# A fused attention and two-layer mixer: TensorE's order inside a slot, the first block sums and the place of w_in's loads

## What is computed

```python
# q, k, v: (2, 8, 768, 64) float32; block 32, window 16
k_sum = k.reshape(B, H, nb, block, D).max(axis=3)
v_sum = v.reshape(B, H, nb, block, D).mean(axis=3)
scores_l = scale * q @ k.T, kept where |i - j| < window, else -1e9
scores_s = scale * q @ k_sum.T + log(block)
a = softmax(concat(scores_l, scores_s))
x = a @ concat(v, v_sum)                 # (2, 768, 512) after the heads are joined
h = relu(x @ w_in); u, v = halves of h; v = layer norm of v
x = (u * (w_spatial @ v + b)) @ w_out    # then the second mixer, with a convolution and a gate
```

## Time and profile before

| | us |
|---|---|
| median of 3 runs | 348.29 |
| lowest, highest | 347.79, 354.48 |
| profiled execution, its own time | 351.07 |
| profiled execution, its span | 349.1 |
| PE busy in the span | 337.3 |

### The profile page before, as it was taken

One profiled execution on the slowest core, in us unless ns is written; L12 is line 12 of the kernel. 1 busy time (PEld: TensorE's weight loads), 2 busy tenths in 40 slices (PEclk: granted clock), 3 DMA queues, 4 the chain that ended last, 5 costly groups with the idle time before them and its releaser, 6 DMA issues.

```text
span 349.1 us, 7117 instructions
## 1 busy us (share of the span) xinstructions
PE 337.3 (97%) x2890; PEld 303.3 (87%) x2890; DVE 211.4 (61%) x503; ACT 123.6 (35%) x364; POOL 117.5 (34%) x130
## 2 busy tenths in 40 slices
PE   8868899999999999999999999999999999999996
PEld 7657788888998899889999999998989999999984
DVE  5656788534308990354446984688656667766652
ACT  3656878656233132351111124231222232222212
POOL 6637768766609999400004930000000000000000
PEclk9989999999999999999999999999999999999999
DMA  8997849000212300163000100000000004000004
GB/s 251 282 262 190 279 112 323 7 2 3 62 60 70 116 11 2 45 200 118 0 0 2 60 0 3 0 2 0 0 2 0 0 2 180 0 2 0 0 3 180
DMA packets 9025, 24.72 MB, mean 71 GB/s; under 512 B 1185, under 2 KB 1185, under 8 KB 8993
## 3 DMA queue, kind: packets, MB, share of 16 engines
q1 hardware_dynamic: 8992, 24.26, 22.8%
HBM read 21.11 MB, written 3.15 MB: 69 GB/s over the span
## 4 chain that ended last, share of the span: by engine, by line
PE 91%; DMA 5%; SPq 2%; issue 1%; DVE 0%; DVEq 0%
PE bank L799 26%; PE bank L801 26%; PE bank L800 26%; PE bank L791 4%; DMA vw<-in_vw 4%; PE bank L778 3%; PE bank L758 3%; PE bank L849 2%; PE bank L768 1%; PE bank L852 1%; SPq L282 1%; DMA out<-obuf 1%; SPq L276 0%; DVE obuf L702 0%; SPq L271 0%
## 5 line engine op out<-in xcount | busy, mean ns | idle before, releaser
L801 PE MATMUL bank<-g_h,W_l 128*128 128x384 f32 x128 | 43.0, 336 | 0.0
L800 PE MATMUL bank<-g_l,W_h 128*128 128x384 f32 x128 | 43.0, 336 | 0.0
L799 PE MATMUL bank<-g_h,W_h 128*128 128x384 f32 x128 | 42.9, 335 | 0.0
L505 ACT ACTIVATE P<-P,nmax 128x120 f32<-128x120 f32 x96 | 36.7, 384 | 15.5 <-DVE nmax L634 15.4
L800 PE MATMUL bank<-wo_l,hg_h 128*128 128x512 f32 x96 | 38.0, 396 | 0.0
L801 PE MATMUL bank<-wo_h,hg_l 128*128 128x512 f32 x96 | 38.0, 396 | 0.0
L799 PE MATMUL bank<-wo_h,hg_h 128*128 128x512 f32 x96 | 38.0, 395 | 0.0
L421 POOL TENSOR_TENSOR P<-P,rinv 128x480 f32<-128x480 f32 x24 | 23.6, 986 | 26.1 <-DVE rinv L622 25.7
L801 PE MATMUL bank<-wsT_h,vn_l 128*128 128x384 f32 x96 | 32.1, 334 | 0.0
L799 PE MATMUL bank<-wsT_h,vn_h 128*128 128x384 f32 x96 | 32.1, 334 | 0.0
L800 PE MATMUL bank<-wsT_l,vn_h 128*128 128x384 f32 x96 | 32.1, 334 | 0.0
(11 more groups left out here) (111 smaller groups left out, 796.6 us busy)
## 6 DMA issues: line engine op xcount, KB each, us to landing
vw<-in_vw SPq DMA_DIRECT2D x16, 288.0 KB, 6.5
kT<-in_k SPq DMA_DIRECT2D x8, 384.0 KB, 5.1
qT<-in_q SPq DMA_DIRECT2D x8, 384.0 KB, 6.2
out<-obuf SPq DMA_DIRECT2D x12, 256.0 KB, 2.0
stage<-in_wsT SPq DMA_DIRECT2D x6, 384.0 KB, 3.1
stage<-in_w SPq DMA_DIRECT2D x4, 512.0 KB, 3.5
stage<-in_wo SPq DMA_DIRECT2D x4, 512.0 KB, 3.6
wi_most<-in_w_in SPq DMA_DIRECT2D x3, 512.0 KB, 12.9
```

The lines of the kernel that those rows point to most:

```text
L505: a.activation(P[:, i % NP_, j, :], P[:, i % NP_, j, :], ACT.Exp, bias=nmax[:, c:c + 1], scale=-1.0, accum_out=rsum[:, c, 0:1]).then_inc(e ...
L799: t_.matmul(dst, lhs[0](c), rhs[0](c), start=first, stop=False)
L800: t_.matmul(dst, lhs[0](c), rhs[1](c), start=False, stop=False)
L801: ins = t_.matmul(dst, lhs[1](c), rhs[0](c), start=False, stop=last)
```

## The change

In each slot, TensorE's transposes and values move ahead of the fills and of the identity transposes; the identity transposes of slot 0 go from 10 to 6. The block sums of pair 0 move one slot forward, "vs" from slot 1 to 0 and "vp" from 2 to 1, and `spread_sums(0)` on GpSimd moves from behind the normalization of item 1 to behind that of item 0. Pair 1 keeps slots 3 and 4, and all later pairs keep theirs. SyncE issues `vw` of a pair ahead of the quarter of w_in, not behind it. The orders on VectorE and ScalarE stay, but for the takes of pair 0's sums, which go with their fills.

```diff
@@ -177,7 +177,7 @@
         for p in range(NP):
-            at = GP * p - 1 if p >= 2 else 2 * p + 1
+            at = GP * p - 1 if p >= 2 else 3 * p
             fills_at[at].append(("vs", p))
             fills_at[at + 1].append(("vp", p))
@@ -298,9 +298,9 @@
             for p in range(NP):
                 load_k(p)
                 load_q(p)
+                load_v(p)
                 if 2 <= p < 2 + KC:
                     load_wi(p - 2)
-                load_v(p)
@@ -388,7 +388,7 @@
-                pool.wait_ge(norm_done, GP * p + 1 if p >= 2 else GP * p + 2)
+                pool.wait_ge(norm_done, GP * p + 2 if p == 1 else GP * p + 1)
@@ -420,7 +420,7 @@
-                if i in (2, 5) or i >= 2 * GP and i % GP == 1:
+                if i in (1, 5) or i >= 2 * GP and i % GP == 1:
                     spread_sums(i // GP)
@@ -880,17 +880,17 @@
             for i in range(SLOTS):
                 if i < NG:
                     scores(i)
+                if 2 <= i < NG + 2:
+                    transpose_probs(i - 2)
+                if 3 <= i < NG + 3:
+                    values(i - 3)
+                for _ in range(6 if i == 0 else 4 if i < 3 else 0 if i > 7 or any(u[0] == "vs" for u in fills_at[i]) else 3):
+                    t_.transpose(bank[1][:, 0:128], ident[:, :], ident[:, :])
                 for u in fills_at[i]:
                     if u[0] == "piece":
                         piece(*u[1:])
                     else:
                         dense(u)
-                for _ in range(10 if i == 0 else 4 if i < 3 else 0 if i > 7 or any(u[0] == "vs" for u in fills_at[i]) else 3):
-                    t_.transpose(bank[1][:, 0:128], ident[:, :], ident[:, :])
-                if 2 <= i < NG + 2:
-                    transpose_probs(i - 2)
-                if 3 <= i < NG + 3:
-                    values(i - 3)
```

## The result

The changed kernel takes 356.15 us (median of 4 runs, 354.83 to 359.3) against 349.0 us for the kernel before: ratio 1.0177, 95% interval 1.0121 to 1.0234. The ratios are estimated from the single executions without the slower state of the chip, so they are not quotients of the medians. It is slower, by 5 to 6 us going by the ratios (the medians lie 7.15 and 4.69 us apart); whether that is more than 2% the intervals leave open. The forecast was slower by 3.35 us, 351.6 us in a range of 347.4 to 354.0. The profiled execution of the changed kernel has a span of 357.3 us against 349.1, and it is one of the longer ones (its own time is 359.3).

A forecast was written before the change was run, and what follows sets the result against it. The prediction took TensorE (PE), 91% of the chain, as the bound. Waits on ACT's copies of 0.7 + 2.0 + 1.55 us less 0.9 in the front gave +3.35 on 348.3: 351.6 us, range 347.4 to 354.0.

The forecast's parts named there:

- the front: Before slot 12: more PE work done ahead of each instruction block boundary, so slot 12 starts 0.9 us earlier.
- ACT's late copy in slots 20, 23 and 26: PE waits for ACT's copy behind a dense tile's take: 1.0 us in slots 20 and 23, 1.55 in 26.
- slots 14 and 17: PE's transposes wait for ACT's copy of the transposed probabilities, 0.35 us in each slot, 0.7 us together.
- The work is the same, only what stands where a block ends differs.: Early slots: reordering leaves PE's work equal and changes only the work left behind the last block boundary, gaining 0.9 us.
- Fetch gaps behind slot 12: From 44 us on PE crosses instruction block boundaries without idle time, so no loss was put there.
- The wait for `vw`: Pair 2's block sums: vw lands about 1.9 us earlier, near 19 us, so the 1.06 us wait goes.
- a start of slot 12 before 42 us: Sign that the reading of instruction fetches setting the front's pace fails; slot 12 was expected near 43.3 us.
- The gaps were forecast longer than before: Front: "issue" gaps stay 124 matmuls apart and grow, as PE does more before each boundary and then stands longer.
- The first sums: Pair 0's sums moved to slot 0: costed at 0, with bounds of 1.25 us gain and 1.0 us loss.
- rival 4: The clock falls at the new waits on ACT: one fall 353.1 us, three (slots 20, 23, 26) 356.1; chance 0.18.
- Rival 3: The waits on ACT do not show because ACT is ahead by then: 347.4 us; chance 0.07.
- Rival 2: The front opens: early fetch gaps vanish and the clock stays high, 345.9 us, or 349.2 for half; chance 0.2.

The follow-up runs named there:

- e5: Changed kernel with the loads of the second layers' weights held until item 19's scores are done: 356.32 us against 351.54 for the kernel before.
- e4: Changed kernel with ScalarE's copy of the transposed probabilities ahead of x_h and, in slots 20, 23, 26, the dense tile's take: 353.77 us, ratio 1.0070 to the kernel before.
- e14: Changed kernel with the second layers' weight loads held back, run once more for a second trace; the traced execution took 357.10 us.
- e12: Kernel before with one more identity transpose ahead of the four transposes of slots 8 to 17: one execution, 351.76 us against 350.52.
- e13: Kernel before with one more identity transpose behind the values of slots 8 to 17, ahead of the next scores: one execution, 353.56 us against 350.52.
- e8: Changed kernel run again, unaltered, beside the kernel before on another chip: 355.94 against 351.25 us, ratio 1.0149.
- e6: Changed kernel with the values moved back to the end of the slot (scores, transposes, fills, values): 349.15 us, ratio 0.9912 to the kernel before.
- e9: Changed kernel with values last in the slot and ScalarE's copy ahead of x_h and the last dense tile: 347.85 us, ratio 0.9894 to the kernel before.
- e11: Same as e10, with the four loads of w_in one pair later (pairs 3 to 6) and its split one step later: 347.75 us, ratio 0.9897 to the kernel before.
- e10: Same as e9, with the first block sums back in slots 1 and 2 and ten identity transposes in slot 0: 347.36 us, ratio 0.9886 to the kernel before.
- e7: Kernel before with only the loads changed, vw ahead of w_in in SyncE's queue: 349.29 us against 351.54, ratio 0.9916.

## Why the prediction failed

**Direction and first cause were right.** The order costs more than the front gives, by ACT's late copy in slots 20, 23 and 26. Forecast 1.0, 1.0 and 1.55 us, measured as idle time 0.85, 0.85 and 1.34. The idle time says a little too little: at slot 20 the transposes start 1.61 us behind the scores, forecast 1.67, and slot 20 takes 6.53 us in e5 and 5.62 in e4, which has no wait, 0.91. In slots 14 and 17 0.35 us each were forecast; e14, which has no gap there, shows 2.86 and 2.85 us against 2.68 for both, 0.18 each. All of ACT's late copies together: forecast 4.25, measured 3.6 us (e5 and e14 against e4).

**The step that failed is the sentence "The work is the same, only what stands where a block ends differs."** The work was the same, but what stands next to what was not: one more change of kind in each slot that ends with a piece or a dense tile and is followed by scores (12, 13, 15, 16, 18 to 22), 0.16 us by e12 and e13. The forecast has no term for it; e4 measures 1.26 us from slot 12 on. The forecast's sum for the late part, 4.25 us, came near the measured 4.85 only by luck, because its waits were 0.65 us too large. So this term alone does not explain the miss. Going by the ratios the loss was 5.2 to 6.2 us, 1.9 to 2.8 over the forecast: 0.6 of it is the late part, 0.7 the front, and the rest fits the fetch gaps behind slot 12. The next two points take up the front and the gaps.

**The front gave next to nothing,** the second term that failed: -0.9 us forecast, -0.2 in the trace after and a start of slot 12 later than before in e8 and e14 (44.94 and 45.48 us). The wait for `vw` went, as forecast, and the next gap took it over. The 0.9 us rested on the blocks arriving when they had; in the seventeen traces of the two kernels and the variants slot 12 starts between 40.45 and 46.14 us: they don't arrive at fixed times. The forecast took a start of slot 12 before 42 us as a sign that fetches do not set the front's pace. It came in four traces (e5, e6, e9, e11), but these have 0 to 2.06 us of fetch gaps in the front against 4.04 before, so it fits fetches that come out differently from one execution to the next and does not speak against them. The gaps were forecast longer than before; in the trace after the front holds 2.85 us of them, and the new waits and the low clock in slot 8 take the difference. The first sums were costed at nothing with a loss of 1.0 us as a bound; they brought a wait of 0.95 us on POOL at 15.78, by `spread_sums(0)` ahead of the second normalization, which the forecast named and priced at nothing. The scores of slot 4 start at 17.77 us, 1.24 later than before, so the delay was not covered by the block awaited at 15.92 us: VectorE's copy, for which `values(0)` waits too, ended at 15.39 there, as this row of the kernel before shows, and that left room for 0.5 us.

```profile
14.70 0.69 DVE L602 COPY pT<-bank 120x512 f32<-120x512 f32 x1 [0.60 <-PE bank L778]
```

The time of e9 and e10 doesn't differ for it.

**Fetch gaps behind slot 12 were put at nothing**, the third term that failed: 1.89 us in the trace after, and with the last of them the clock fell, which costs 0.5 us in slot 17 (sums 1.33 us against 0.79) and about 1.0 in slot 18 (5.37 against 4.22 with 0.15 of it for the change of kind). That is rival 4 by another cause: the clock fell behind a fetch gap, not behind the waits on ACT, which left it at 1.00 in every trace. That the fetches cost nothing after 44 us was read from one execution of the kernel before. Why the new order has gaps there is open; e5 and e14 point at the loads that are in flight.

**The range** ended at 354.0 us for reasons that add up: the three terms above; and the base, whose median was 348.3 in the first three runs, 349.0 beside the result and 350.8 to 351.5 later, so that the forecast on the time itself, and not on the ratio, was 0.7 us low in the comparison of the result and 2.5 to 3.3 in the later ones. The ratio forecast was 1.0096; the interval begins at 1.0121, or at 1.0097 in the second comparison.

Rival 3 (the waits don't show) is refuted by six traces. Rival 2 (the front opens) is seen in single executions: e5's front is 3.8 us shorter than before.

## What to carry to other kernels

Where one engine is busy throughout, an order that keeps the work equal can still change its price: count how often neighbouring instructions change kind, and read the length of the loop body, since "busy" hides it. Moving a consumer forward takes away the cover of the producer behind it; here, moving the producer forward too (e4) took 3.6 us off slots 12 on. Set against the kernel before, even the best variants win next to nothing in these slots (0.2 us); their 1.1% lies in the front. And a difference of a few microseconds between two single traces may be instruction fetches that come out differently next time; compare stretches that don't hold any, and look for a packet of the instruction queue some 2.6 us before the gap's end.

## What the hardware showed that was not expected

- A change of kind costs time without idle time: an identity transpose of 128 x 128 takes 0.11 us beside transposes and 0.25 us between values (120 x 64) and scores (64 x 64 tiles).
- PE's program comes in blocks of about 125 matmuls, and PE has stood up to 2.67 us for one (e7, with a DMA share of 1.00 in the gap); a gap ends 2.3 to 2.9 us behind the start of a packet on the instruction queue; the same program showed the three early gaps as 0 in one execution and as 0.99, 2.52 and 2.27 us in another. The Trainium skill (Runtime: NRT & Kernel Launch, Instruction fetch mechanics) calls this mostly hidden; in the front of this kernel the measurement disagrees.
- The clock does not follow the longest gap. One of 1.60 us at slot 17 was followed by a granted clock of 0.52; in e14, gaps of 2.52 and 2.27 us were followed by 1.00, in the columns of the earlier trace rows:

```profile
31.40:35.00 3.60, 3.53 (x87) 2.83 (x91) 1.83 (x10) 2.50 (x10) 1.50 (x2) 1.00 0.27 78
44.60:48.00 3.40, 3.30 (x76) 2.79 (x77) 1.69 (x10) 1.92 (x9) 0.17 (x1) 1.00 0.55 160
```

What decides it isn't shown by these runs.
